# The mean square of x spread by TensorE, the inverse root taken by GpSimd on 512 columns

## What is computed

```python
a = softmax(normalised(k).T @ normalised(q) / tau)          # 256 x 256
x = v @ a
rms = np.sqrt(np.mean(x * x, axis=-1, keepdims=True) + 1e-06)
xn = x / rms * rms_g
g = xn @ w_gate
y = (g * sigmoid(g) * (xn @ w_val)) @ w_out
out = (sigmoid(y @ w2_gate) * (y @ w2_val)) @ w2_out
```

## Time and profile before

| | |
|---|---|
| median of 3 runs | 1309.59 us (1308.84 to 1310.41) |
| span of the profiled execution | 1307.8 us |
| mean granted clock of TensorE | 0.999 of full speed |
| TensorE | 1295.0 us busy, 99% |
| VectorE | 655.3 us, 50% |
| ScalarE | 455.3 us, 35% |
| GpSimd | 37.7 us, 3% |

### The profile page before, as it was taken

How to read it: one execution, slowest core, us unless ns; L and a number is a source line. 1 busy time by engine, 2 the same in 40 slices (tenths; PEclk the granted TensorE clock), 3 DMA queues, 4 the chain that set the end, 5 groups by cost and what they waited for, 6 DMA issues and landing times.

```text
span 1307.8 us, 15519 instructions
## 1 busy us (share of the span) xinstructions
PE 1295.0 (99%) x5706; PEld 1067.3 (82%) x5706; DVE 655.3 (50%) x1014; ACT 455.3 (35%) x737; POOL 37.7 (3%) x32
## 2 busy tenths in 40 slices
PE   8999999999999999999999999999999999999998
PEld 7878888888888888888888888888888888889888
DVE  6776544544554554554454455455455455445333
ACT  5453533333332333333333333333333333333322
POOL 0000500000000000000000000000000000000000
PEclk9999999999999999999999999999999999999999
DMA  9910000100100100010010010010010001000000
GB/s 345 315 57 1 1 1 1 33 0 0 32 0 0 32 0 0 8 24 0 0 32 0 0 32 0 0 32 0 0 25 7 0 0 28 1 1 17 1 17 13
DMA packets 60569, 34.43 MB, mean 26 GB/s; under 512 B 50816, under 2 KB 54144, under 8 KB 60544
## 3 DMA queue, kind: packets, MB, share of 16 engines
q1 hardware_dynamic: 60544, 34.09, 8.9%
HBM read 27.92 MB, written 6.16 MB: 26 GB/s over the span
## 4 chain that ended last, share of the span: by engine, by line
PE 98%; DVE 1%; DMA 0%; SPq 0%; POOL 0%; issue 0%; ACT 0%; DVEq 0%
PE ps L661 21%; PE ps L662 21%; PE ps L663 21%; PE ps L779 10%; PE ps L780 10%; PE ps L781 10%; PE ps L727 3%; PE ps L687 1%; DMA qk<-in_k 0%; PE ps L696 0%; PE ps L703 0%; SPq L250 0%; POOL small L296 0%; PE ps L713 0%; DVE w_lo_v L442 0%
## 5 line engine op out<-in xcount | busy, mean ns | idle before, releaser
L596 DVE TENSOR_TENSOR h<-ps,h 128x512 f32<-128x512 f32 (+1 forms) x288 | 196.1, 681 | 328.0 <-PE ps L663 322.2
L390 ACT ACTIVATE h_hi<-h 128x512 fp32r<-128x512 f32 (+1 forms) x288 | 179.6, 624 | 406.9 <-DVE h L596 405.3
L384 ACT ACTIVATE h<-ps 128x512 f32<-128x512 f32 (+1 forms) x288 | 169.9, 590 | 402.5 <-PE ps L663 402.5
L601 DVE TENSOR_TENSOR h_lo<-h,h_hi 128x512 fp32r<-128x512 f32 (+1 forms) x288 | 195.4, 679 | 131.0 <-ACT h_hi L390 127.1
L779 PE MATMUL ps<-h_hi,w_hi_o 128*128 128x512 f32 (+1 forms) x576 | 225.9, 392 | 0.0
L780 PE MATMUL ps<-h_lo,w_hi_o 128*128 128x512 f32 (+1 forms) x576 | 225.8, 392 | 0.0
L781 PE MATMUL ps<-h_hi,w_lo_o 128*128 128x512 f32 (+1 forms) x576 | 225.3, 391 | 0.0
L592 DVE TENSOR_TENSOR h<-ps,h 128x512 f32<-128x512 f32 (+1 forms) x144 | 98.0, 681 | 165.5 <-ACT h L384 164.8
L781 PEld LDWEIGHTS ps<-h_hi,w_lo_o 128*128 128x128 f32 x576 | 110.8, 192 | 23.0
L779 PEld LDWEIGHTS ps<-h_hi,w_hi_o 128*128 128x128 f32 x576 | 110.2, 191 | 23.6
L780 PEld LDWEIGHTS ps<-h_lo,w_hi_o 128*128 128x128 f32 x576 | 110.1, 191 | 21.9
(11 more groups left out here) (111 smaller groups left out, 1321.6 us busy)
## 6 DMA issues: line engine op xcount, KB each, us to landing
v_in<-in_v SPq DMA_DIRECT2D x44, 128.0 KB, 3.2
out<-out_sb SPq DMA_DIRECT2D x44, 128.0 KB, 2.6
qk<-in_q SPq DMA_DIRECT2D x10, 512.0 KB, 7.6
qk<-in_k SPq DMA_DIRECT2D x10, 512.0 KB, 9.1
w_raw_g<-in_moe_w_gate SPq DMA_DIRECT2D x6, 512.0 KB, 7.9
w_raw_v<-in_moe_w_val SPq DMA_DIRECT2D x6, 512.0 KB, 8.0
w_raw_o<-in_moe_w_out SPq DMA_DIRECT2D x6, 512.0 KB, 9.0
qk<-in_q SPq DMA_DIRECT2D x3, 256.0 KB, 2.9
```

The source lines that it names most:

```text
L384: nc.scalar.activation(h[:, slot, 0:w], ps[:, GATE[slot], 0:w], ACT.Sigmoid).then_inc(sig_done, 1)
L390: nc.scalar.activation(h_hi[:, part, 0:w], h[:, slot, 0:w], ACT.Copy).then_inc(hi_done, 1)
L596: nc.vector.tensor_tensor(h[:, slot, 0:w], ps[:, VALUE[slot], 0:w], h[:, slot, 0:w], ALU.mult).then_inc(h_done, 1)
L601: nc.vector.tensor_tensor(h_lo[:, part, 0:w], h[:, slot, 0:w], h_hi[:, part, 0:w].bitcast(F32), ALU.subtract).then_inc(lo_done, 1)
```

## The change

For blocks 1 to 11 the sums, the small power, the diagonals and the spread are replaced. The sum of squares (128x512) is split into a high and a low part, and a 128x128 matrix filled with 1/256 is multiplied by both: two matmuls give the mean square, already on all partitions. ScalarE copies it out of PSUM and adds 1e-6; POOL raises all 128x512 values to -0.5; VectorE multiplies x by the result from SBUF. The stations move: both splits of v to tile 0, `make_x` after step 1, squares and gains to tile 2, the split of the squares to tile 3, `spread_mean` after step 4, the copy at tile 5, `x_norm` at tile 9, both `xs_low` at tile 10. Block 0 keeps the old way. The `keep_warm` products before the first layer get other operands and widths.

```diff
-            def inverse_rms(b):
-                w = width(b)
-                pool.wait_ge(ms_ready, b + 1)
-                nc.gpsimd.tensor_tensor(rinv[:, 0:w // P], ms[:, 0:w // P], halves[:, 1, 0:w // P], ALU.pow)\
-                  .then_inc(rinv_done, 1)
+                w = width(b)
+                pool.wait_ge(ms_copied, b)
+                if not (isinstance(b, int) and b == 1):
+                    pool.wait_ge(xn_done, b * 2)
+                nc.gpsimd.tensor_tensor(rinv_all[:, 0:w], sq[:, 0, 0:w], halves[:, 1, 0:1].broadcast_to([P, w]), ALU.pow)\
+                  .then_inc(rinv_all_done, 1)
...
+            def squares_high(b, dst):
+
+                w = width(b)
+                act.wait_ge(squares_added, b)
+                nc.scalar.activation(dst[0][:, 0, 0:w], sq[:, 0, 0:w], ACT.Copy).then_inc(sq_hi_done, 1)
+
+            def mean_copy(b):
+
+                w = width(b)
+                act.wait_ge(ms_spread, b)
+                nc.scalar.activation(sq[:, 0, 0:w], ps[:, X[0], 0:w], ACT.Copy, bias=1e-6).then_inc(ms_copied, 1)
...
-                mid[1] = [(vt_high, b, c, vt) for c in range(CC)]
-                mid[3] = [(x_square, b, c) for c in range(CC)]
+                mid[0] = [(vt_high, b, c, vt) for c in range(CC)]
+                mid[2] = [(x_square, b, c) for c in range(CC)]
+                mid[3] = [(squares_high, b, vt)]
+                mid[5] = [(mean_copy, b)]
...
+            def squares_low(b, dst):
+
+                w = width(b)
+                dve.wait_ge(sq_hi_done, b)
+                nc.vector.tensor_tensor(dst[1][:, 0, 0:w], sq[:, 0, 0:w], dst[0][:, 0, 0:w].bitcast(F32), ALU.subtract)\
+                  .then_inc(sq_lo_done, 1)
+
             def x_norm(b, c):
                 w = width(b)
-                dve.wait_ge(rinv_spread, b + 1)
+                if isinstance(b, int) and b == 0:
+                    dve.wait_ge(rinv_spread, 1)
+                    by = ps[:, X[1], 0:w]
+                else:
+                    dve.wait_ge(rinv_all_done, b)
+                    by = rinv_all[:, 0:w]
...
+            nc.vector.tensor_scalar(mean_r[:, :], ones[:, :], 1.0 / C, None, ALU.mult).then_inc(mean_r_done, 1)
...
-                for j, work in {0: [(turn_v, b, 0), (turn_v, b, 1)],
-                                1: [(vt_low, b, 0, vt), (vt_low, b, 1, vt)],
-                                3: [(x_gain, b, 0), (x_gain, b, 1), (add_squares, b)],
-                                5: [(mean_square, b)],
-                                6: [(diagonal, b, vt)],
-                                8: [(x_norm, b, 0), (x_norm, b, 1)]}.items():
+                for j, work in {0: [(turn_v, b, 0), (turn_v, b, 1), (vt_low, b, 0, vt), (vt_low, b, 1, vt)],
+                                2: [(x_gain, b, 0), (x_gain, b, 1), (add_squares, b)],
+                                3: [(squares_low, b, vt)],
+                                9: [(x_norm, b, 0), (x_norm, b, 1)]}.items():
...
-                        extras[9] = [(xs_low, b + 2, 0)]
-                        extras[10] = [(xs_low, b + 2, 1)]
+                        extras[10] = [(xs_low, b + 2, c) for c in range(CC)]
...
+            def spread_mean(b, squares):
+
+                w = width(b)
+                if isinstance(b, int) and b == 1:
+                    pe.wait_ge(mean_r_done, 1)
+                pe.wait_ge(xg_done, b * 2 + 1)
+                pe.wait_ge(sq_hi_done, b)
+                nc.tensor.matmul(ps[:, X[0], 0:w], mean_r[:, :], squares[0][:, 0, 0:w], start=True, stop=False)
+                pe.wait_ge(sq_lo_done, b)
+                nc.tensor.matmul(ps[:, X[0], 0:w], mean_r[:, :], squares[1][:, 0, 0:w], start=False, stop=True)\
+                  .then_inc(ms_spread, 1)
...
-            def keep_warm(n):
-
-                for _ in range(n):
-                    nc.tensor.matmul(ps[:, Y[1], 0:JG * P], w_hi["g1"][:, 0, 0:P], w_hi["g1"][:, 0, 0:JG * P],
+            def keep_warm(n, weights, moving):
+
+                for i in range(n):
+                    nc.tensor.matmul(ps[:, Y[1], 0:moving.shape[-1]], weights[i % len(weights)], moving,
                                      start=True, stop=True)
...
-            keep_warm(18)
+            pe.wait_ge(vt_hi_done, 1)
+            keep_warm(18, gate_tiles, xs[0][:, 0, 0:480])
             pe.wait_ge(a_lo_done, CC)
             make_x(0, xs)
-            keep_warm(6)
+            keep_warm(6, gate_tiles[:1], w_hi["g1"][:, 0, 0:JG * P])
             sum_squares(0)
             pe.wait_ge(ones_r_done, 1)
-            keep_warm(10)
+            keep_warm(10, gate_tiles, a_flat[:, 0:448])
             spread_rms(0, xs)
-            keep_warm(12)
+            keep_warm(12, gate_tiles, a_flat[:, 0:496])
...
-                    if j == 2:
+                    if j == 1:
                         make_x(b, vt)
                     if j == 4:
-                        sum_squares(b)
-                    if j == 7:
-                        spread_rms(b, vt)
+                        spread_mean(b, vt)
```

More of the change, by code:

```diff
@@ L119, in build @@
         ones_r = sb("ones_r", [P, P], F32R)
+        mean_r = sb("mean_r", [P, P], F32R)
         rinv_hi = sb("rinv_hi", [P, 4], F32R)
@@ L125, in build @@
         small = sb("small", [P, 64])
+        rinv_all = sb("rinv_all", [P, BLOCK])
         a_hi = sb("a_hi", [P, CC, C], F32R)
@@ L181, in build @@
         diag_done, rinv_spread, xn_done = sem("diag_done"), sem("rinv_spread"), sem("xn_done")
+        mean_r_done, sq_hi_done, sq_lo_done = sem("mean_r_done"), sem("sq_hi_done"), sem("sq_lo_done")
+        ms_spread, ms_copied, rinv_all_done = sem("ms_spread"), sem("ms_copied"), sem("rinv_all_done")
         xs_hi_done, xs_lo_done = sem("xs_hi_done"), sem("xs_lo_done")
@@ L291, in _ @@
             nc.gpsimd.tensor_tensor(norm, ssq, halves[:, 0, :], ALU.pow).then_inc(norm_ready, 1)
+            pool.wait_ge(ms_ready, 1)
+            nc.gpsimd.tensor_tensor(rinv[:, 0:BLOCK // P], ms[:, 0:BLOCK // P], halves[:, 1, 0:BLOCK // P], ALU.pow)\
+              .then_inc(rinv_done, 1)
             def inverse_rms(b):
                 w = width(b)
-                pool.wait_ge(ms_ready, b + 1)
-                nc.gpsimd.tensor_tensor(rinv[:, 0:w // P], ms[:, 0:w // P], halves[:, 1, 0:w // P], ALU.pow)\
-                  .then_inc(rinv_done, 1)
-            for b in range(2):
-                inverse_rms(b)
+                pool.wait_ge(ms_copied, b)
[3 more added lines that the diff above has]
+                  .then_inc(rinv_all_done, 1)
+            inverse_rms(1)
             for n, (w, g) in enumerate(SPLITS_2):
@@ L512, in diagonal @@
                                             ALU.mult).then_inc(diag_done, 1)
+            def squares_low(b, dst):
[3 more added lines that the diff above has]
+                  .then_inc(sq_lo_done, 1)
             def x_norm(b, c):
                 w = width(b)
-                dve.wait_ge(rinv_spread, b + 1)
+                if isinstance(b, int) and b == 0:
[4 more added lines that the diff above has]
+                    by = rinv_all[:, 0:w]
                 dve.wait_ge(xg_done, b * 2 + c + 1)
-                nc.vector.tensor_tensor(x_raw[:, c, 0:w], x_raw[:, c, 0:w], ps[:, X[1], 0:w], ALU.mult)\
-                  .then_inc(xn_done, 1)
+                nc.vector.tensor_tensor(x_raw[:, c, 0:w], x_raw[:, c, 0:w], by, ALU.mult).then_inc(xn_done, 1)
             def xs_low(b, c):
@@ L675, in sum_squares @@
                 nt = width(b) // P
[L678 to L684, removed]
+                pe.wait_ge(x_squared, CC)
+                pe.wait_ge(xg_done, 1)
                 for n in range(nt):
-                    for c in range(chunks_left):
+                    for c in range(CC):
                         mm = nc.tensor.matmul(ps[:, X[0], n:n + 1], sq[:, c, n * P:(n + 1) * P], ones[:, 0:1],
-                                              start=(c == 0), stop=(c == chunks_left - 1))
+                                              start=(c == 0), stop=(c == CC - 1))
                 mm.then_inc(ms_made, 1)
+            def spread_mean(b, squares):
[8 more added lines that the diff above has]
+                  .then_inc(ms_spread, 1)
             def spread_rms(b, diag):
@@ L698, in spread_rms @@
                 mm.then_inc(rinv_spread, 1)
-            def keep_warm(n):
-                for _ in range(n):
-                    nc.tensor.matmul(ps[:, Y[1], 0:JG * P], w_hi["g1"][:, 0, 0:P], w_hi["g1"][:, 0, 0:JG * P],
+            def keep_warm(n, weights, moving):
+                for i in range(n):
+                    nc.tensor.matmul(ps[:, Y[1], 0:moving.shape[-1]], weights[i % len(weights)], moving,
                                      start=True, stop=True)
+            gate_tiles = [w_hi["g1"][:, 0, j * P:(j + 1) * P] for j in range(JG)]
+            a_flat = a_hi[:, :, :].rearrange("p c m -> p (c m)")
             def column_norms():
```

## The result

The changed kernel takes 1963.82 us (median, 1962.92 to 1964.75) against 1309.74: a ratio of 1.4993 (95% interval 1.4975 to 1.501). The forecast was 1301.9. Rival (1), at some 1930 us, is what happened. The profiled execution has a span of 1962.5 us, 654.7 more than before.

What follows compares the result with a forecast made beforehand. TensorE's back-to-back matmuls bound the kernel: 1307.8 - 9.45 (sums) - 0.1 (start-up) + 1.8 (first layer) = 1300.1 us of span, so 1301.9 us median with the power hidden. Likeliest range 1299.5 to 1304, reaching to 1320.

Steps and rivals of the forecast that it cites:

- Rival (1): GpSimd's power costs 81 us by its columns, stalling every block: 630 us more, about 1930 us; chance 0.18.
- What the 512-column power costs: GpSimd's power between 1.2 and 81 us; 10 us taken as likeliest, hidden in about three cases of four.
- the argument for overlap: GpSimd's power: columns may overlap, as unrolling hides dependent fp32 latency; 81 us would become 10 to 20.
- The rest of the path, from a late power to TensorE's wait: Steady blocks: x_norm, two xs_high, h_hi and h_lo follow a late power, 3.3 us; past 22 us, one for one.
- What is removed: TensorE, blocks 1 to 11: dropping the sums of squares saves 0.88 us a block, 9.45 us together.
- What is added: TensorE: two spread_mean products replace the two of spread_rms, same number, width and kind: nothing added.
- Start-up: keep_warm bursts before the first layer: the last 12 shrink to 496 columns, gaining 0.1 us.
- The first layer: Block 0: moved steps meet VectorE's weight splits, TensorE loses 1.8 us, bounded by 0.9 and 2.8.
- The dates: Steady blocks: the power has 17.9 us before anyone waits, 22 us before TensorE does; other moves covered.
- Sum: Whole kernel: 1307.8 - 9.45 - 0.1 + 1.8 = 1300.1 us of span.
- The power's growth beside VectorE: GpSimd and VectorE meeting in SBUF: a 10 us power grows by 2 us at most.
- Rival (4): Steady blocks: POOL's long SBUF use holds up VectorE, 5.7 us late each block, about 1360 us; chance 0.03.

Runs made afterwards that it cites:

- experiment 1: The changed kernel with GpSimd's power replaced by a subtraction of the same shape, so x is scaled by wrong numbers: 1301.85 us, ratio 0.9939.
- the doses: The changed kernel with the power on only the first 128, 144 or 160 columns and a subtraction on the others: 1302.42, 1332.84 and 1373.78 us.
- experiment 12: Kernel with a 16-column power and stations at the dates of the kernel before, plus an unused 128-byte-a-partition tile behind its two new tiles: 1299.56 us, ratio 0.9927.
- experiment 7: The changed kernel with the power taken on 16 columns between two VectorE turns, ScalarE's copy dropped: 1297.73 us, ratio 0.9906.
- experiment 3: The changed kernel with the power on 144 columns and a subtraction on the other 368: 1332.84 us, ratio 1.0177.

## Why the prediction was wrong

The step that failed is in "What the 512-column power costs": "I take the geometric middle, 10 us, as likeliest, with 20 well inside its error, and hold it hidden in about three cases of four". The only rows of that operation gave 81 us, and 81.92 was measured. The lower end came from another operation, a subtraction. Between these ends the nearest row is the one of the same operation; the middle of the two stood for nothing. Rival (1) should have been the forecast, and the argument for overlap, which no row showed, a rival. The rest of the path, from a late power to TensorE's wait, was right.

The Trainium skill (GPSIMD Engine Reference, Performance pitfalls for Q7 kernels) has unrolling hide the latency of a dependent chain. I leaned on it as if the power were written that way. The trace doesn't show it for this operation: from 3 to 4 columns, at 128 and at 512 the price is 0.16 us a column.

The other steps, against experiment 1 and the doses:

- **What is removed** (0.88 us a block): right, 105.27 - 104.39 = 0.88. The two new tiles of the changed kernel in front of a_hi take 512 and 2048 bytes a partition, ten times 256. If only the place within 256 bytes counts, as experiment 12 suggests, the place has no part in this difference. With the unused tile in both kernels it is 104.86 - 103.93 = 0.93.
- **What is added**: nothing, right.
- **Start-up** (0.1 us): the first up product started at 68.07, before at 68.16; right in this pair of profiles, though the start differs by up to 1 us from one profile to another.
- **The first layer** (1.8 us): 1.6 us, 87.30 - 85.68. Right.
- **The dates** (VectorE from 17.9 us on, TensorE from 22): right. 128 columns, 20.7 + 0.8 us, made VectorE wait 3.8 us and cost nothing, so VectorE's date is 17.7; the other doses give 22.2 for TensorE. The prediction put 36 matmuls at 8.2 us; two of its own steps of 4.22 make 8.4, and with that its sum gives the 22.2 too.
- **Sum** (1300.1 us of span): 1300.0 with the subtraction.
- **The power's growth beside VectorE** (2 us at most on 10): the reading was incomplete, and the term too large. The 1.01 us power at 200.04 had an `h_lo` beside it too, from 200.59 on. What the powers that took longer share is an instruction under way at their start (experiment 7), and 81.92 us show no growth.
- **Rival (4)**, VectorE held up by GpSimd: excluded. In the first 18 us of a power, 427 to 445 us, VectorE's `h_lo` takes 693 ns, as in the earlier trace rows:

```profile
L637 DVE TENSOR_TENSOR h_lo<-h,h_hi 128x512 fp32r<-128x512 f32 x4 | 2.8, 693 | 2.8 <-ACT h_hi L412 2.8
```

Rival (1)'s price was 630 us of waits; they are 634.8. It lacked the half clock. The sum of the changed kernel is 1300.0 + 634.8 = 1934.8, and 27.7 us are left to 1962.5. Of these, 22.2 came back when TensorE was kept busy in ten of the eleven waits. Added up from the rows behind each wait, what the matmuls take beyond their pace at full clock (0.234 us for 512 columns, 0.18 for 384) comes to some 26 us: 23.6 behind those ten and 2.4 behind the first layer's, which no run filled. Some 2 us stay open.

## What to carry to other kernels

Price an operation from rows of that operation, even at another size, and take its slope at its word; overlap that no row shows is a rival. Where a value stands on many partitions, ask whether a costly operation can be done on fewer copies: 16 columns and two turns did what 512 columns did, in 3.3 us of GpSimd for 82. A wait can cost more than itself when it stops TensorE: here even 1.95 us of idle time brought eight or nine matmuls at half clock behind it in four cases of nine.

## What was not expected of the hardware

TensorE's pace depends on where tiles lie in SBUF. Moving a_hi and all behind it by 128 bytes a partition takes 0.41 us off a block of the kernel before and 0.46 off the changed one with the subtraction (some 450 matmuls, so 1 ns each); 256 bytes, tried in one kernel, give it back. It is worth 4 to 5 us of 1300, half as much as the sums of squares that the change removed. Which pair of tiles it is, weights or moving data, was not tried.

The half clock doesn't come behind every wait, and not always at once. In the kernel with 144 columns the wait in front of 445.67 left the pace at 0.23 us, while an equally long one brought the slow matmuls of experiment 3:

```profile
445.67 0.51 PE L827 MATMUL ps<-h_hi,w_hi_o 128*128 128x512 f32 x1 [1.94 <-DVE h_lo L641]
446.01 0.39 PE L828 MATMUL ps<-h_lo,w_hi_o 128*128 128x512 f32 x1
```

In the kernel with 240 unread products a wait of 3.52 us ended at 1012.38 with matmuls at full clock, and those at half clock began 1 us later, some 0.43 us apart until 1016.84:

```profile
1012.38 0.51 PE L823 MATMUL ps<-h_hi,w_hi_o 128*128 128x512 f32 x1 [3.52 <-DVE h_lo L637]
...
1013.43 0.62 PE L824 MATMUL ps<-h_lo,w_hi_o 128*128 128x512 f32 x1
1013.86 0.63 PE L825 MATMUL ps<-h_hi,w_lo_o 128*128 128x512 f32 x1
```

What decides between these cases, no run here shows.
